# A fused attention and two feed-forward layers on one core: the first four pairs' sums and inverses begun by ScalarE, with new orders of work

## The reference

```python
scores = scale * np.matmul(q, k.transpose(0, 1, 3, 2))
scores = np.where(mask, scores, -1000000000.0)
scores = scores - np.max(scores, axis=-1, keepdims=True)
attn = np.exp(scores)
attn = attn / (np.sum(attn, axis=-1, keepdims=True) + 1e-09)
x = np.matmul(attn, v)
```

## Time and profile before

| | |
|---|---|
| median of 3 runs | 913.8 us (912.16 to 915.25) |
| the profiled execution's own time | 916.3 us |
| its span in the trace | 914.5 us |
| PE busy | 894.1 us, 98% |
| DVE, ACT, POOL busy | 501.6, 501.5, 203.1 us |
| DMA | 58.31 MB, q1 (begun by SP) 23.1% of 16 engines' span |

### The profile page before, as it was taken

How to read it: one execution, slowest core, us unless ns; L and a number is a source line. 1 busy time by engine, 2 the same in 40 slices (tenths; PEclk the granted TensorE clock), 3 DMA queues, 4 the chain that set the end, 5 groups by cost and what they waited for, 6 DMA issues and landing times.

```text
span 914.5 us, 15361 instructions
## 1 busy us (share of the span) xinstructions
PE 894.1 (98%) x5609; PEld 828.6 (91%) x5609; DVE 501.6 (55%) x1008; ACT 501.5 (55%) x996; POOL 203.1 (22%) x198
## 2 busy tenths in 40 slices
PE   8987999999999999999999999999999999999997
PEld 6765999999999999999999999999989899999996
DVE  4456883553635445431113588576576576576564
ACT  3545764544535454431222688566566566566664
POOL 8544352443433425211444000000000000000000
PEclk9989999999999999999999999999999999999999
DMA  5866523323222222201410600200200200200000
GB/s 132 193 149 149 159 70 86 69 70 94 58 79 66 73 77 68 61 14 54 170 61 8 237 1 1 70 1 1 69 0 0 69 0 0 69 0 0 35 1 35
DMA packets 53077, 58.31 MB, mean 64 GB/s; under 512 B 26145, under 2 KB 36618, under 8 KB 53018
## 3 DMA queue, kind: packets, MB, share of 16 engines
q1 hardware_dynamic: 52874, 57.45, 23.1%
q10 hardware_dynamic: 144, 0.07, 0.0%
HBM read 38.34 MB, written 9.51 MB: 52 GB/s over the span
## 4 chain that ended last, share of the span: by engine, by line
PE 78%; ACT 4%; DVE 3%; issue 1%; POOL 0%; POOLq 0%; ACTq 0%; DVEq 0%
PE M_ps L696 8%; PE M_ps L698 7%; PE M_ps L697 7%; PE S_ps L785 4%; PE S_ps L784 4%; PE S_ps L783 4%; PE O_ps L761 3%; PE O_ps L759 3%; PE O_ps L760 3%; PE M_ps L761 3%; PE M_ps L759 3%; PE M_ps L760 3%; PE M_ps L706 3%; PE M_ps L708 3%; PE M_ps L707 3%; PE T_ps L784 2%
## 5 line engine op out<-in xcount | busy, mean ns | idle before, releaser
L696 PE MATMUL M_ps<-x,w_h 128*128 128x288 f32 x576 | 172.0, 299 | 1.5 <-DVE x L844 1.2
L697 PE MATMUL M_ps<-x,w_l 128*128 128x288 f32 x576 | 169.6, 294 | 0.0
L698 PE MATMUL M_ps<-x,w_h 128*128 128x288 f32 x576 | 169.6, 294 | 0.0
L696 PEld LDWEIGHTS M_ps<-x,w_h 128*128 128x128 f32 x576 | 108.1, 188 | 3.5 <-DVE x L844 1.4
L816 DVE TENSOR_REDUCE neg_max<-S_ps 128x1 f32<-128x192 f32 (+4 forms) x160 | 71.0, 482 | 73.4 <-PE S_ps L600 73.3
L697 PEld LDWEIGHTS M_ps<-x,w_l 128*128 128x128 f32 x576 | 108.2, 188 | 0.1
L698 PEld LDWEIGHTS M_ps<-x,w_h 128*128 128x128 f32 x576 | 108.1, 188 | 0.0
L1105 ACT ACTIVATE away<-rest 128x384 f32<-128x384 f32 x96 | 50.5, 526 | 98.8 <-DVE rest L925 98.8
L1199 POOL TENSOR_TENSOR h_l<-h_f,h_h 128x288 fp32r<-128x288 f32 x48 | 39.7, 827 | 223.1 <-ACT h_h L1043 223.1
L855 DVE TENSOR_TENSOR m_tmp<-M_ps,m_tmp 128x288 f32<-128x288 f32 x48 | 21.9, 456 | 118.5 <-PE M_ps L698 118.4
L1025 ACT ACTIVATE pt_h<-T_ps 128x448 fp32r<-128x448 f32 (+1 forms) x88 | 44.1, 502 | 74.5 <-PE T_ps L646 74.0
(11 more groups left out here) (120 smaller groups left out, 2270.3 us busy)
## 6 DMA issues: line engine op xcount, KB each, us to landing
qk_hl<-qk_hm SPq DMA_DIRECT2D x64, 144.0 KB, 2.4
qk_raw<-qT SPq DMA_DIRECT2D x32, 144.0 KB, 3.0
qk_raw<-kT SPq DMA_DIRECT2D x32, 144.0 KB, 3.1
w_raw<-w SPq DMA_DIRECT2D x12, 384.0 KB, 5.1
inv_b<-inv_d SPq DMA_DIRECT2D x16, 288.0 KB, 3.9
y_d<-y_out SPq DMA_DIRECT2D x32, 144.0 KB, 1.8
y_raw<-y_d SPq DMA_DIRECT2D x6, 768.0 KB, 4.8
out<-o_out SPq DMA_DIRECT2D x18, 256.0 KB, 2.2
```

Of the source, the lines that this page charges most:

```text
L696: mm(o, w_h, x_h, start=k == 0, stop=False)
L697: mm(o, w_l, x_h, start=False, stop=False)
L698: last = mm(o, w_h, x_l, start=False, stop=k == KM - 1)
```

## The change

Five things.

1. For the pairs of items 0 to 7 (`BY_ACT_LAST`), the transfers `sum`, `inv_out`, `inv_in` are begun by ACT in place of SP, with the same waits; they go through ACT's own DMA queue. In the bare periods `sum` has a lag of 2 and not 3: it stands right behind `take` of the same period.
2. ACT's bare order puts `take` and `sum` ahead of the exponential `x4`; the weights' high parts are made between `x3` and `m`, and one piece or more a period earlier than before. DVE's low parts follow a table of their own, `W_LOW`.
3. PE's bare order: `x1` before `s0`, `x3` before `s4`, `vB` between `s4` and `m`. PE's full order: `vB` before `s1`.
4. SP's orders: without the three steps in bare periods; in full periods `copy_q` comes earlier, `sum` later, `copy_k` behind all weights' loads as before.
5. ACT's single wait for `x_lowed` comes seven groups later, just ahead of its first split of a weight of `w_in`.

```diff
-LAG = {"full": LAG, "bare": dict(LAG, sum=3, norm0=6, norm1=5, norm_high=5, norm_low=5)}
+LAG = {"full": LAG, "bare": dict(LAG, norm0=6, norm1=5, norm_high=5, norm_low=5)}
...
-    "bare": ["s1", "s0", "x1", "vA", "x2", "s4", "x3", "fill", "x4", "m", "vB", "vC", "vD"],
+    "bare": ["s1", "x1", "s0", "vA", "x2", "x3", "s4", "vB", "fill", "x4", "m", "vC", "vD"],
...
-    "bare": ["W1", "x1", "x2", "x3", "m", "x4", "W2", "norm_high", "take"],
+    "bare": ["x1", "x2", "inv_in", "x3", "W1", "m", "inv_out", "norm_high", "take", "sum", "x4", "inv_soon"],
...
-    "bare": ["load", "copy_k", "W1", "sum", "copy_q", "W2", "load_v", "inv_out", "m", "inv_soon", "inv_in"],
-    "full": ["inv_in", "load", "G1", "sum", "inv_out", "copy_q", "W1", "load_v", "W2", "copy_k", "G3", "m", "G2"],
+    "bare": ["load", "copy_k", "W1", "m", "copy_q", "load_v", "W2"],
+    "full": ["inv_in", "load", "G1", "copy_q", "inv_out", "load_v", "W1", "W2", "copy_k", "sum", "m", "G3", "G2"],
...
-W_SPLIT = {8: (0,), 9: (1, 2), 10: (3, 4, 5), 11: (6, 7, 8, 9, 10), 12: (11, 12, 13, 14, 15, 16),
+W_SPLIT = {7: (0,), 8: (1,), 9: (2, 3, 4), 10: (5, 6, 7), 11: (8, 9, 10, 11), 12: (12, 13, 14, 15, 16),
            13: (17, 18, 19, 20, 21, 22, 23)}
+W_LOW = {8: (0,), 9: (1,), 10: (2, 3, 4), 11: (5, 6, 7, 8, 9), 12: (10, 11, 12, 13, 14, 15, 16),
+         13: (17, 18, 19, 20, 21, 22, 23)}
...
+            def sum_in(n):
+                pair = n // 2
+                act.wait_ge(o_taken, n + 1)
+                act.dma_start(*sums_of(pair)).then_inc(sum_loaded[pair % 2], 16)
+
+            def inv_out(n):
+                pair = n // 2
+                act.wait_ge(inverted, pair + 1)
+                act.dma_start(*inverses_of(pair)).then_inc(inv_stored, 16)
+
+            def inv_in(n):
+                pair = n // 2
+                act.wait_ge(inv_stored, 16 * (pair + 1))
+                if pair >= 1:
+                    act.wait_ge(x_normed, 2 * pair)
+                act.dma_start(*rows_of(pair)).then_inc(inv_loaded[pair % 2], 16)
...
-            act.wait_ge(x_lowed, N_MAIN // 2)
             for g in range(G_FIRST[N_PERIODS], N_GROUPS):
                 if g == HIDDEN_EARLY:
                     whole_turns(0, 0)
                 group(g)
+                if of_last(g) == W_IN_SPLIT[0]:
+
+                    act.wait_ge(x_lowed, N_MAIN // 2)
```

More of the change, by code:

```diff
@@ L88 @@
        "inv_in": 4, "norm0": 5, "norm1": 4, "norm_high": 4, "norm_low": 4, "split": -1, "load": -1, "load_v": 0, "split_v": 1}
-FIRST_LAST = H - 1
+BY_ACT_LAST = H - 1
 LAG["inv_soon"] = 3
-LAG = {"full": LAG, "bare": dict(LAG, sum=3, norm0=6, norm1=5, norm_high=5, norm_low=5)}
+LAG = {"full": LAG, "bare": dict(LAG, norm0=6, norm1=5, norm_high=5, norm_low=5)}
 PE_PERIOD = {
-    "bare": ["s1", "s0", "x1", "vA", "x2", "s4", "x3", "fill", "x4", "m", "vB", "vC", "vD"],
-    "full": ["vA", "s1", "vB", "s0", "x1", "x2", "vC", "vD", "G1", "x3", "s4", "G3", "x4", "m", "G2"],
+    "bare": ["s1", "x1", "s0", "vA", "x2", "x3", "s4", "vB", "fill", "x4", "m", "vC", "vD"],
+    "full": ["vA", "vB", "s1", "s0", "x1", "x2", "vC", "vD", "G1", "x3", "s4", "G3", "x4", "m", "G2"],
 }
 DVE_PERIOD = {
-    "bare": ["s1", "s0", "norm1", "s4", "inv", "norm0", "x1", "x2", "x3", "x4", "W1", "norm_low", "W2"],
+    "bare": ["s1", "s0", "norm1", "s4", "inv", "norm0", "W1", "norm_low"],
     "full": ["s0", "inv", "norm1", "norm0", "x1", "s1", "norm_low", "G1", "x2", "s4", "x3", "G3", "W1", "G2",
@@ L102 @@
 ACT_PERIOD = {
-    "bare": ["W1", "x1", "x2", "x3", "m", "x4", "W2", "norm_high", "take"],
-    "full": ["W1", "x1", "x2", "norm_high", "take", "G1", "x3", "split", "G3", "m", "x4", "W2", "G2"],
+    "bare": ["x1", "x2", "inv_in", "x3", "W1", "m", "inv_out", "norm_high", "take", "sum", "x4", "inv_soon"],
+    "full": ["x1", "x2", "norm_high", "W1", "take", "G1", "x3", "split", "G3", "m", "x4", "W2", "G2"],
 }
@@ L410, in pt_of, with sums_of, inverses_of, rows_of @@
             return pt[n % 2 if n < ROOMY else 0]
+        def sums_of(pair):
+            return sums[0:D, pair % 2, :], o_f[D:D + 1, 2 * (pair % 2):2 * (pair % 2) + 2, :]
+        def inverses_of(pair):
+            return inv_d[pair, :].rearrange("(p c) -> p c", p=D), inv_sum[0:D, pair % 2, :]
+        def rows_of(pair):
+            return inv_b[0:D, :], inv_d[pair:pair + 1, :].partition_broadcast(D)
         def of_last(g):
@@ L473, in sum_in @@
                 sp.wait_ge(o_taken, n + 1)
-                sp.dma_start(sums[0:D, pair % 2, :], o_f[D:D + 1, n % 4 - 1:n % 4 + 1, :]).then_inc(sum_loaded[pair % 2], 16)
+                sp.dma_start(*sums_of(pair)).then_inc(sum_loaded[pair % 2], 16)
             def inv_out(n):
@@ L478, in inv_out @@
                 sp.wait_ge(inverted, pair + 1)
-                sp.dma_start(inv_d[pair, :].rearrange("(p c) -> p c", p=D), inv_sum[0:D, pair % 2, :]).then_inc(inv_stored, 16)
+                sp.dma_start(*inverses_of(pair)).then_inc(inv_stored, 16)
             def inv_in(n):
@@ L483, in inv_in @@
                 sp.wait_ge(inv_stored, 16 * (pair + 1))
-                if pair >= 1:
-                    sp.wait_ge(x_normed, 2 * pair)
-                sp.dma_start(inv_b[0:D, :], inv_d[pair:pair + 1, :].partition_broadcast(D)).then_inc(inv_loaded[pair % 2], 16)
+                sp.wait_ge(x_normed, 2 * pair)
+                sp.dma_start(*rows_of(pair)).then_inc(inv_loaded[pair % 2], 16)
             def store_y(g):
@@ L504, in step @@
                     maxima(n)
-                elif name == "sum" and n % 2:
+                elif name == "sum" and n % 2 and n > BY_ACT_LAST:
                     sum_in(n)
-                elif name == "inv_out" and n % 2:
+                elif name == "inv_out" and n % 2 and n > BY_ACT_LAST:
                     inv_out(n)
-                elif (name == "inv_in" and n % 2 and n != FIRST_LAST) or (name == "inv_soon" and n == FIRST_LAST):
+                elif name == "inv_in" and n % 2 and n > BY_ACT_LAST:
                     inv_in(n)
@@ L895, in _ @@
                                 value, None, ALU.mult).then_inc(rows_set, 1)
-            walk(step, DVE_PERIOD, W_SPLIT)
+            walk(step, DVE_PERIOD, W_LOW)
             for g in range(G_FIRST[N_PERIODS], N_GROUPS):
@@ L1072, in step @@
                     normalise_high(n)
+                elif name == "sum" and n % 2 and n <= BY_ACT_LAST:
+                    sum_in(n)
+                elif name == "inv_out" and n % 2 and n <= BY_ACT_LAST:
+                    inv_out(n)
+                elif (name == "inv_in" and n % 2 and n < BY_ACT_LAST) or (name == "inv_soon" and n == BY_ACT_LAST):
+                    inv_in(n)
                 elif name == "weights":
```

## The result

The changed kernel takes **918.52 us** (median of 20 runs, 915.98 to 923.48) where the kernel before, on the same chips, takes 915.45 (20 runs, 912.16 to 919.31). The ratio is **1.0035, interval 1.0021 to 1.0049**: slower by 3 us, where I forecast 6 us less. The prediction was wrong in its sign.

What follows compares the result with a forecast made beforehand. PE waited for `take` behind sums and inverses queued in SP's DMA queue, and the clock fell: 13.6 us too many in periods 6 to 10. Terms 8.6 - 1.4 - 1.8 + 0.6 = 6.0 gave a median of 907.8 us, range 902 to 912.5.

Steps and rivals of the forecast that it cites:

- Group 0, period 11: Group 0's fourth block needs pair 3's inverses, landing 4.6 behind `vA` instead of 3.2: 1.4 us lost, idle 1.16 becomes 2.6.
- `copy_k`, 0.6: SP's full periods: one `copy_q` less ahead of `copy_k` at 111.47, so the idle 1.47 shrinks by 0.6 us.
- my 6.0 of gain: Whole kernel: all terms summed, 8.6 - 1.4 - 1.8 + 0.6 = 6.0 us faster; this forecast's chance 0.50.
- The stretch: Periods 6 to 10, from 39.94 to period 11's first `vA`: 43.7 us become 35.1, a gain of 8.6.
- my 2 to 3.5: Sums begun by ACT on its own queue: they land in 2 to 3.5 us.
- my tolerance of 4.2: Bare periods: up to 4.2 us of latency of the sums does no harm, DVE's 1.4 being done in time.
- rival D: ACT's in-order list waits for `inverted` ahead of `take`, three waits of 3.4 us: +4.8, 918.6 us; chance 0.08.
- my "about 75": Sign of being right: no PE gap over 1 us from 40 us to period 11's `vA`, at about 75 us.
- The clock: PE's clock behind group 0's longer gap: lowered, charged 1.8 us, bounds 0 to 3.4.
- The 1.75 at the end of attention: PE's gap in period 35, hanging on ACT's wait for DVE's `h_f` at 421.05: stays unchanged.
- the moved wait for `x_lowed`: ACT's later wait, behind its wait for `h_f`: zero effect.
- C: Rival: bytes share 16 engines, what the sums gain `copy_q` loses; gain 1.5 us, 912.3, no change; chance 0.14.

Runs made afterwards that it cites:

- e9: e5 with the weight loads of periods 3 to 10 moved forward to periods 1 to 9, period 11's left in place: 910.18 us, ratio 0.9945.
- e11: The changed kernel with the weight loads of periods 3 to 10 moved forward to periods 1 to 9, period 11's left in place: 918.39 us, ratio 1.0037.
- e3: The changed kernel with all sums and inverses begun by SP again, the other new orders kept: 915.87 us, ratio 0.9998.
- e10: The kernel before with only the weight loads of periods 3 to 10 moved forward to periods 1 to 9: 912.61 us, ratio 0.9979.
- e1: The changed kernel with SP's old order of full periods, sum ahead of copy_q and the weight loads: 915.55 us, ratio 0.9989.
- e4: The kernel before with ACT beginning the twelve transfers, sum right behind take and the later x_lowed wait; other orders as before: 913.94 us, ratio 0.9975.
- e5: The changed kernel with SP's old order of full periods and DVE's norm0 ahead of inv: 913.26 us, ratio 0.9972.
- e6: e4 with DVE's norm0 ahead of inv: 914.08 us, ratio 0.9969.
- e12: The changed kernel with one wait added: SP begins period 11's weight loads only when pair 3's inverses have landed: 916.52 us, ratio 0.9997.
- e2: The changed kernel with DVE's norm0 ahead of inv in bare periods: 915.81 us, ratio 1.0004.
- e7: e4 with SP's new order of full periods, one line apart from it: 918.85 us, ratio 1.0025.
- e8: The changed kernel with twenty filler products on PE just ahead of group 0: 920.56 us, ratio 1.0032.

## Why the prediction was wrong

**The step that failed is "Group 0, period 11".** I took store 1.7 and read 3.9, both from rows of before in which SP stood still, and let the idle 1.16 become 2.6. Store and read took 4.0 and 6.6, the idle became 4.20. The two have causes of their own. The store took 2.9 to 4.7 in the kernels in which ACT begins it, also with SP's old order, and came down to 1.7 and 2.2 only in e9 and e11, where period 10 has no loads of weights; where SP begins it, behind its own wait for the inverses, it took 1.7 (before, e3, e10). That wait went with the first part of the change. The read is what the line of SP's full order costs: 3.5 to 3.8 with the old order or the guard (e1, e4, e5, e6, e12), 5.2 to 6.6 with the new (the changed kernel, e2, e7, e8, e11). I knew that SP's orders change and costed them at `copy_k`, 0.6, alone; I never asked what SP would send at the moment when it no longer waited. The rows that I used for a price were valid only under a wait that the change removes. The time from `vA` to the fourth block rose by 4.6 where I had 1.4: the gain of the stretch, given back at once. Between my 6.0 of gain and the 0.7 of loss in the trace lie 6.7 us: 3.2 of them here, 4.7 in the stretch below, and 1.2 the other way behind the block.

**The stretch: mechanism right, size off.** I forecast 43.7 to 35.1. From the `s1` at 41.15 to `vA` at 79.75 it took 38.6, and a new gap of 1.08 ahead of it (at 36.22, pair 0's) made that `s1` 1.2 later: 3.9 gained, not 8.6, and in e1, e8 and e12, which do the same up to 77 us, 1.5 to 2.4. Two sizes failed. The four sums by ACT landed in 4.6, 4.1, 4.1 and 3.5 us, not in my 2 to 3.5; the three of the stretch lie inside my tolerance of 4.2, pair 0's does not. ACT then waited for `inverted` ahead of its store and `take`, as rival D has it, and that is the new gap of 1.08, in ACT's timeline:

```profile
35.43 0.65 ACT L1047 ACTIVATE o_f<-O_ps 65x576 f32<-65x576 f32 x1 [1.58 <-DVE inv_sum L839]
```

And the tolerance was too wide, because it was reckoned to `inverted`. Behind `inv` on DVE stands `norm0`, and `norm_high` waits for that. DVE's and POOL's timelines of the changed kernel:

```profile
46.98 0.26 DVE L839 RECIPROCAL inv_sum<-sum_eps 64x18 f32<-64x18 f32 x1
47.16 1.85 DVE L851 TENSOR_TENSOR x_f<-o_f,inv_b 64x576 f32<-64x576 f32 x1
```

```profile
46.99 1.41 POOL L1206 TENSOR_TENSOR qk_hl<-qk_raw,qk_hm 64x576 fp32r<-64x576 f32 x1
```

In the stretch `norm0` takes 1.85, 1.85 and 1.83 where it took 0.69 alone at 48.55 before, each time with POOL's L1206 begun 0.17 ahead of it. The Trainium skill, "SBUF — State Buffer", section "SBUF: two separate sides", says that a VectorE operation with two inputs in SBUF and a GpSimd operation that reads SBUF take turns at one pair of ports, and the second waits for the whole of the first. The trace agrees: POOL ends at 48.40, and 0.69 behind that is 49.09, against a measured end of 49.01. The kernel before had it too, in DVE's timeline, with POOL's L1167 begun at 80.22, and I had not used it:

```profile
80.39 1.84 DVE L837 TENSOR_TENSOR x_f<-o_f,inv_b 64x576 f32<-64x576 f32 x1
```

Such a row is a wait as well as work. e2 tests the place: with `norm0` ahead of `inv` it takes 0.74 to 1.07, the gaps of 1.58 and 1.66 fall to 0.43 and 0.80, and `vA` comes at 75.19 for my "about 75".

**The latency beside a full q1.** My prediction had two rules of one page here (the Trainium skill, "DMA: Bandwidth & Descriptors"). By rings that are served in turn the sums pass q1's queue; by "Issuing engines are not separate DMA queues" only the time of issue is saved. Latencies of each pair, us to landing, sums + store + read:

| pair | before (SP) | changed (ACT) |
|---|---|---|
| 0 | 2.2 + 1.8 + 6.2 | 4.6 + 4.2 + 3.9 |
| 1 | 6.1 + 1.7 + 5.1 | 4.1 + 2.3 + 3.5 |
| 2 | 1.8 + 1.7 + 8.0 | 4.1 + 3.0 + 5.4 |
| 3 | 7.0 + 1.7 + 4.0 | 3.5 + 4.0 + 6.6 |
| all | 47.3 | 49.2 |

I had looked at the two sums of 6.1 and 7.0 only. Those became shorter, the other two longer, and the twelve transfers together took no less. Nor was ACT's queue the faster one at the same place: pair 1's sums took 4.1 to 5.8 us in the eleven kernels in which ACT begins them, and 5.1, 5.3 and 6.1 in e10, e3 and the kernel before, where SP does. All twelve stores that SP began in those three took 1.7 to 2.0, the 44 that ACT began 1.7 to 5.3. For 288 KB the sharing is most of it: 3.5 quiet, 6.6 with q1 at 101%. So the runs do not show that a queue of its own passes q1; they do not contradict the second rule.

**The clock.** I charged 1.8 and named the place rightly: 0.83 from 80 to 100 us. I had not seen that half of it begins behind the 3.12 ahead of `vA`. An estimate from the windows: PE was busy for 15.80 us there, at 0.83, and for 17.15 at 0.98 before, which is 2.7 us lost for 0.3; the size was about right. What the clock costs by itself stays open, since e8 failed to fill the gap.

**Right.** The 1.75 at the end of attention is unchanged, the moved wait for `x_lowed` costs nothing, a bare period without a wait did not grow (34.00 - 28.09 = 5.91, for 6.01), and the gap that I had put down to `copy_k` shrank (1.09 at 116.79, for 1.47). The last is no proof of the 0.6: `copy_k` began 1.7 later than before (113.19 for 111.47) where the fourth block was 0.8 later, and the trace puts the gap down to the transfer of the maxima begun behind it.

**The rivals.** D gave 918.6, the median measured, by luck: its +4.8 was counted from 913.8, and the kernel before has its median at 915.45. Its mechanism was there for pair 0 alone, at 1.08 us; its three waits of 3.4 did not come (the gaps are 1.58, 1.66 and 3.12). Its condition, sums past 4.2, is nearer than this trace says: pair 1's took 5.6, 5.1 and 5.2 in e1, e8 and e12. C, that what one transfer gains another loses on shared engines, is nearest in kind, though what lost was not `copy_q` but pair 3's own inverses. The 8 and 14 in a hundred of D and C together were too little: neither of my slower cases asked which traffic a freed queue brings forward.

**Still open.** Why the median lies 1.5 above the profiled execution. Slower executions of the changed kernel show a lower mean clock (0.984 at a span of 921.7, 0.995 at 914.4); over its 20 executions the mean clock is 0.9911, over the 104 of the kernel before beside the experiments 0.9936. On 917 us that would be some 2.3 us (an estimate from these two means), most of the 3.1; together with the sister kernels' later `vA` it suggests gaps that vary from execution to execution. That is argued, not shown. Open is also what in e4 gains: the sums of pairs 1 and 3 and pair 2's read, which the gaps before hung on, are shorter in it (4.6, 4.1 and 4.8 for 6.1, 7.0 and 8.0), but nearly so in e10, where SP begins them (5.1, 3.9 and 6.2). And open is how far the harm of SP's line is the weights alone: e12 holds them back and e1 reorders them, but both move `copy_k` too, and period 11's loads were never moved out of it by themselves.

## What to carry to other kernels

A queue that waits in order is also a brake on its own traffic. Before taking its waits away, list what it will send in the freed time and which critical transfer shares the engines with that; here one line of order turned 0.9975 into 1.0025. Before counting the slow transfers that a change will shorten, list the fast ones that it may lengthen. Take the duration of a transfer only from rows in which the other queues do what they will do after the change, and follow a tolerance to the last instruction that stands behind the awaited one on its engine, not to the awaited one.

## What was unexpected of the hardware

- A queue of its own did not make a 4.5 KB transfer quick beside a busy q1. In the changed kernel, with a DMA share of 0.71 from 40 to 60 us and 0.91 from 60 to 80, sums by ACT took 3.5 to 4.6 us and the stores 2.3 to 4.2; the stores that SP began, in the kernel before, e3 and e10, took 1.7 to 2.0.
- A 64x576 product on DVE takes 1.85 us instead of 0.69 when it starts just behind a POOL operation on SBUF, and DVE's share of busy time hides it: the wait is counted as busy.
- Idles of the same length did and did not cost clock. In the changed kernel the four products behind the idle 1.58 at 50.41 took 1.51 us (clock 0.83 from 50 to 60 us), and the same four behind the idle 1.66 at 65.60 took 0.84 (clock 1.00 from 60 to 80 us). In e12 an idle 1.65 at 66.61 did cost, 1.51 for the four. The length of one gap does not foretell it.
